# Keys and values of the first batch group loaded with 128 tokens on the partitions, and one order of work for all head pairs

## The chip, the cores and the metric

The kernel runs on one core of one Trainium2 chip. The metric is the device time of one execution in microseconds (us); lower is better. The engines are named as the profile names them: PE is TensorE (PEld its weight loads), DVE is VectorE, ACT is ScalarE, POOL is GpSimd, SP is SyncE, which here only issues DMAs (SPq; ACTq is the DMA queue of ACT).

## What is computed

Linear attention over 4 batches of 8 heads, 576 tokens, 64 columns, then two feed-forward layers over the 2304 tokens. Cut from the reference:

```python
kv = np.einsum('bhsd,bhse->bhde', k, v)          # [4, 8, 64, 64], a sum over all 576 tokens
out = np.einsum('bhsd,bhde->bhse', q, kv)
rms = np.sqrt(np.mean(out * out, axis=-1, keepdims=True) + 1e-06)
x = out / rms * g_norm                            # as [2304, 512]
h = x @ w_in;  g = h / (1 + exp(-h));  x = g @ w_out        # 512 -> 2048 -> 512
a = x @ w_a;   b = x @ w_b;            y = (a * b) @ w_out2 # 512 -> 1536 -> 512
```

Since `kv` is a sum over tokens, the order in which tokens lie on partitions does not matter to it, as long as keys and values have the same order.

## The kernel before

Every matrix product of the feed-forward layers is made of three products of split operands (high by high, low by high, high by low), and the up-projection saves products by sums of operands. These layers fill PE from about 38 us on. The change is in what stands ahead of them: the attention of the first **group** (G = 0, batches 0 and 1). The second group's attention (G = 1) is strewn into the feed-forward work, step by step, and is not changed.

The first group is worked off in four **head pairs** h = 0..3 (heads 2h and 2h+1, both batches). For each pair there is one buffer `kvq[h]` of 128 partitions with three planes: keys, values, queries. Before, the keys and the values of a pair come in one DMA each (`heads`, line 292): partitions 0 to 63 hold head 2h and 64 to 127 head 2h+1, each partition nine consecutive tokens, so that one packet is 9*64*4 = 2304 bytes. The queries come in two DMAs (`queries`, line 298), one for each batch, also 2304 bytes a packet. SP issues keys and batch 0's queries, ACT values and batch 1's queries, pair after pair, then each half of the first weight block, `raw_half`.

The stages of one pair, by name:

- `kv(0, h)` (line 695) waits for keys and values and multiplies them into two PSUM banks, nine steps t, each with 64 rows by 64 columns, four such products side by side in the array (two heads, two batches). ACT copies the result to `kv_sb` (`kv_keep`).
- POOL's `turned` (line 616) reorders the queries into `q_tiles` in three copies; `q_turn` (line 715) on PE transposes them, in three thirds j; DVE's `qT_keep` (line 1321) copies each third to `qT_sb`.
- `q_kv` (line 727) multiplies them with `kv_sb`, in three thirds.
- ACT squares each third, DVE sums (`sums`), ACT takes the root (one for the pair, after all three thirds), DVE inverts it (`invert`) and multiplies (`normalise`, line 1338) into `o_sb`.
- `o_turn` (line 742) on PE transposes `o_sb`; ACT's `keep` writes it to `xy`, from which the feed-forward operands are made.

Each engine works off its own list in the order of the program text, with semaphores between them; nothing else sets the order. `plain(0)` (line 1013) is the first feed-forward step on PE. Before the first pair, `warm` (line 985) multiplies zeros that nobody reads, `WARM[0]` times ahead of `kv(0, 0)` and `WARM[1]` times behind it. SP loads the second group's first pair (`load_heads(0)`) into buffer 0 and then weights (`load_raw`) when the last pair's queries have landed.

Of the kernel before, what the change touches and what calls it, by code (L numbers as in the profile page):

```python
# [11 lines left out]
P = 128  # L12
# [3 lines left out]
def fused_attention_ffn_kernel(nc, q, k, v, g_norm, w_in, w_out, w_a, w_b, w_out2, out):  # L16
# [11 lines left out]
    PART = SEQ // 2  # L28
    GTOK = 2 * SEQ
    TILE3 = 3 * P  # L30
    JS = ROWS // 3
    UNITS = PAIRS * JS
    assert KT == 4 and ROWS % 3 == 0 and SEQ == 2 * PART and PART <= 512


    SEGS = [(g, layer) for layer in (1, 2) for g in range(GROUPS)]
# [62 lines left out]
    with ExitStack() as ctx:  # L99
# [189 lines left out]

            return 2 * pp % G_HALVES == G_HALVES - 1  # L290

        def heads(G, h, which):


            dst = kvq[staged(G, h)[0]][:, which, :].rearrange("p (b e) -> p b e", b=2)
            return dst, (k, v)[which][2 * G:2 * G + 2, 2 * h:2 * h + 2].rearrange("b h (p t) d -> (h p) b (t d)", t=ROWS)

        def queries(h, bb):

            dst = kvq[h][bb * HALF:(bb + 1) * HALF, 2, :].rearrange("p (h e) -> p h e", h=2)  # L300
            return dst, q[bb, 2 * h:2 * h + 2].rearrange("h (p t) d -> p h (t d)", t=ROWS)

        def head_by_tiles(h, bb, odd):

# [18 lines left out]
        def last_quarter(half, c):  # L323
# [5 lines left out]
        def staged(G, h):  # L329

            return (0, h + 2) if G else (h, 1)

        def units(at, steps):

# [95 lines left out]
        @block.sync  # L430
        def _(sp):
            def raw_free(r):

                n = max(n for n in range(len(SEGS)) if RAW0[n] <= r)
                layer = SEGS[n][1]
                p, what = divmod(r - RAW0[n], layer + 1)
                if what == layer:
                    sp.wait_ge(d_ready, 2 * (PAIR0[n] + p + 1))
                elif p < PLAIN_PAIRS and n == 0:
                    sp.wait_ge(w_ready, RING * (p + 1))  # L440
                else:
                    sp.wait_ge(w_sum, sums_before(PROD0[n] + layer * p + what + 1, 4))

            def load_raw(r):
                n = max(n for n in range(len(SEGS)) if RAW0[n] <= r)
                layer = SEGS[n][1]
                p, what = divmod(r - RAW0[n], layer + 1)
                if r >= RAWS:
                    raw_free(r - RAWS)
                dst = raw[:, r % RAWS, :]  # L450
                cols = slice(2 * p * P, 2 * (p + 1) * P)
                if what == layer:
                    w = w_out if layer == 1 else w_out2
                    dst, src = dst.rearrange("p (f n) -> p f n", f=2), w[cols, :].rearrange("(f p) n -> p f n", p=P)
                else:
                    w = w_in if layer == 1 else (w_a, w_b)[what]
                    dst = dst.rearrange("p (c n) -> p c n", c=KT)
                    src = w.rearrange("(c p) n -> p c n", p=P)[:, :, cols]
                sp.dma_start(dst, src).then_inc(raw_in[r % RAWS], 16)

            def load_heads(h):


                before = PAIRS + h - 1 if h else 0
                sp.wait_ge(kv_mm, before + 1)
                sp.wait_ge(qT_mm, JS * (before + 1))
                for which in range(2):
                    sp.dma_start(*heads(1, h, which)).then_inc(kv_in[0], 16)
# [12 lines left out]
            sp.dma_start(*raw_half(0)).then_inc(raw_in[0], 16)  # L481

            sp.wait_ge(q_in[PAIRS - 1], 32)
            load_heads(0)
            load_raw(1)
            for r in range(2, RAW0[-1]):
                load_raw(r)
                if r == 2:
                    load_heads(1)
                if r == 5:  # L490
                    load_heads(2)
                if r == 8:
                    load_heads(3)
                if r == RAW0[3] + 5:
                    sp.wait_ge(flushed, DOWN0[3])
                    for j in range(TOK_TILES):
                        for half in range(2):
                            sp.dma_start(*half_tile(0, j, half)).then_inc(stored, 16)

            for j in range(TOK_TILES - 1):  # L500
                sp.wait_ge(flushed, down0(PAIR0[-1] - 1) + j + 1)
                sp.dma_start(*half_tile(1, j, 0)).then_inc(stored, 16)
            for c in range(2):
                sp.wait_ge(flushed, DOWN0[-1] + c)
                sp.dma_start(*last_quarter(0, c)).then_inc(stored, 16)
            sp.wait_ge(stored, 16 * (2 * GROUPS * TOK_TILES + 2))
# [180 lines left out]
        def _(pe):  # L687
# [6 lines left out]

            def kv(G, h):

                buf, fill = staged(G, h)
                b0, b1 = BANK_D, BANK_D + 1
                pe.wait_ge(kv_in[buf], 32 * fill)
                if (G, h) == (0, 1):  # L700
                    pe.wait_ge(kv_kept2, 1)
                wait_turn(b0)
                wait_turn(b1)
                for t in range(ROWS):
                    for odd, bank in enumerate((b0, b1)):
                        rows = slice(odd * HALF, odd * HALF + HD)
                        for bb in range(2):
                            cols = slice(bb * SEQ + t * HD, bb * SEQ + (t + 1) * HD)
                            mm = pe.matmul(ps[bb * HALF:(bb + 1) * HALF, bank, 0:HD],  # L709
                                           kvq[buf][rows, 0, cols], kvq[buf][rows, 1, cols],  # L710
                                           start=(t == 0), stop=(t == ROWS - 1))
                mm.then_inc(kv_mm, 1)
                turn[b0] = turn[b1] = (kv_kept, PAIRS * G + h + 1)

# [269 lines left out]

            def warm(count):
                for _ in range(count):

                    zeros = wt[:, 0:2, :].rearrange("p a n -> p (a n)")
                    pe.matmul(ps[:, first_bank(1, 0), :], ident[:], zeros, start=True, stop=True)  # L989

            pe.wait_ge(consts, 3)
            pe.wait_ge(cleared, 1)
            warm(WARM[0])
            kv(0, 0)
            warm(WARM[1])
# [1 line left out]
                q_turn(0, 0, j, first_bank(0, j))  # L997
            for h in range(PAIRS):
                for j in range(JS):
                    if h > 1:  # L1000
                        o_turn(0, h - 1, j, result_bank(h - 1, j))
                    q_kv(0, h, j, prod_bank(h, j))
                if h + 1 < PAIRS:

                    kv(0, h + 1)
                    for j in range(JS):
                        if h == 0:

                            o_turn(0, 0, j, result_bank(0, j))
                        q_turn(0, h + 1, j, first_bank(h + 1, j))  # L1010

            pe.wait_ge(x_kept, UNITS - JS)
# [21 lines left out]
        def _(act):  # L1034
# [30 lines left out]
            def kv_keep(G, h):  # L1065
                n = PAIRS * G + h
                act.wait_ge(kv_mm, n + 1)
                if n >= 2:
                    act.wait_ge(o_mm, JS * (n - 1))
                act.wait_ge(cleared, 2)  # L1070
                for odd, bank in enumerate((BANK_D, BANK_D + 1)):
                    if n == 0 and odd:

# [203 lines left out]
            kv_keep(0, 0)  # L1277
            for h in range(PAIRS):
                for j in range(JS):
                    if h > 1:  # L1280
# [4 lines left out]
                root(0, h)  # L1285
                if h + 1 < PAIRS:
                    kv_keep(0, h + 1)
                if h == 0:
                    for j in range(JS):
                        keep(0, 0, j, result_bank(0, j))  # L1290
                if h in (1, 2):
                    half_round(0, h - 1)
                    half_round(7, h - 1)
# [20 lines left out]

        @block.vector
        def _(dve):
            nc.vector.memset(wt[:, 0:2, :], 0.0).then_inc(cleared, 1)
            nc.vector.memset(kv_sb[:], 0.0).then_inc(cleared, 1)
            dve.wait_ge(cleared, 2)

            def qT_keep(G, h, j, bank):
                i = UNITS * G + JS * h + j
# [361 lines left out]
            for h in range(PAIRS):  # L1684
# [2 lines left out]
                invert(0, h)  # L1687
                for j in range(JS):
                    normalise(0, h, j)
                    if 0 < h < PAIRS - 1:  # L1690
                        qT_keep(0, h + 1, j, first_bank(h + 1, j))
                if h == 0:

                    for j in range(JS):
                        qT_keep(0, 1, j, first_bank(1, j))
            first_pair()
            second_pair()
            for pp in range(2, PAIR0[-1]):
# [36 lines left out]
```

## Time and profile before

| | us |
|---|---|
| median of 3 runs | 870.26 |
| the three runs | 870.24, 870.26, 873.62 |
| the profiled execution | 873.04 |
| its span in the profile | 871.2 |

The profile is one execution. Its span is the time from the first to the last instruction on the core; 1.8 us of that execution's own time lie outside it. Times in the trace count from the span's start. The share of an engine's busy time in the span says how full it is; the chain of waits follows back what released the last instruction, step by step, and so says which work set the end. In the table of windows the granted clock of PE is 1.00 for 2.4 GHz and 0.50 for 1.2 GHz.

### The profile page before, as it was taken

The numbers are of one execution on the slowest core, as the hardware profiler recorded it, in microseconds if no ns is written. First come the engines' busy times: TensorE is split into PE (matmuls) and PEld (weight loads), VectorE is DVE, ScalarE is ACT, GpSimd is POOL, SyncE is SP. The second block draws the span as 40 slices with busy tenths as digits, with TensorE's granted clock in tenths as the row PEclk, the third lists the DMA queues.
The fourth block names the chain that finished last, engine by engine and source line by source line (L and its number), as shares of the span: only waits on it lengthen the run. The fifth ranks groups of instructions, "written<-read, shape, count | busy, mean of one in ns | idle before, by whom it ended". The sixth has DMA issues, their size and how long they took to land.

```text
span 871.2 us, 16097 instructions
## 1 busy us (share of the span) xinstructions
PE 860.4 (99%) x6208; PEld 813.8 (93%) x6208; DVE 510.6 (59%) x776; ACT 279.0 (32%) x465; POOL 610.1 (70%) x889
## 2 busy tenths in 40 slices
PE   8899999999999999999999999999999999999998
PEld 5699999999999999999999999999999999999997
DVE  4665656757886666665765355364484553544636
ACT  3764434534543323222532122121242211212210
POOL 2566545666578777766778697797889876877760
PEclk9999999999999999999999999999999999999999
DMA  9664123111011111111101111021011330210104
GB/s 300 158 156 106 49 57 75 50 49 49 26 49 49 46 28 50 50 49 49 49 25 49 50 49 49 25 63 60 25 49 49 109 98 25 74 49 25 49 25 109
DMA packets 47002, 55.56 MB, mean 64 GB/s; under 512 B 11728, under 2 KB 32464, under 8 KB 46928
## 3 DMA queue, kind: packets, MB, share of 16 engines
q1 hardware_dynamic: 44192, 49.55, 19.9%
q10 hardware_dynamic: 2736, 4.98, 1.8%
q8 instruction: 51, 0.84, 0.4%
q14 instruction: 23, 0.19, 0.1%
HBM read 49.81 MB, written 4.72 MB: 63 GB/s over the span
## 4 chain that ended last, share of the span: by engine, by line
PE 98%; DVE 1%; issue 1%; ACT 0%; POOL 0%; POOLq 0%
PE ps L777 49%; PE ps L863 8%; PE ps L864 8%; PE ps L865 8%; PE ps L885 6%; PE ps L887 6%; PE ps L886 6%; PE ps L794 3%; PE ps L737 2%; PE ps L747 1%; PE ps L989 1%; PE ps L709 1%; PE ps L723 1%; DVE o_sb L1350 0%; DVE stat L1331 0%
## 5 line engine op out<-in xcount | busy, mean ns | idle before, releaser
L777 PE MATMUL ps<-x_hi,w_hi 128*128 128x288 f32 x1064 | 229.8, 297 | 0.5 <-issue 0.3
L777 PE MATMUL ps<-x_lo,w_hi 128*128 128x288 f32 x1064 | 228.1, 296 | 0.0
L777 PE MATMUL ps<-x_hi,w_lo 128*128 128x288 f32 x1064 | 226.8, 295 | 0.0
L777 PEld LDWEIGHTS ps<-x_hi,w_hi 128*128 128x128 f32 x1064 | 179.0, 188 | 13.7 <-issue 5.1
L777 PEld LDWEIGHTS ps<-x_hi,w_lo 128*128 128x128 f32 x1064 | 171.7, 189 | 0.0
L777 PEld LDWEIGHTS ps<-x_lo,w_hi 128*128 128x128 f32 x1064 | 169.9, 188 | 0.0
L1142 ACT COPY kept<-ps 128x576 f32<-128x576 f32 x114 | 73.2, 642 | 288.1 <-PE ps L777 287.6
L523 POOL TENSOR_SCALAR w_hi<-wt 128x256 fp32r<-128x256 f32 x152 | 69.9, 460 | 123.4 <-PE ps L777 116.4
L1473 DVE TENSOR_TENSOR xy<-xy,ps 128x384 f32<-128x384 f32 (+1 forms) x188 | 94.0, 510 | 89.0 <-PE ps L865 88.7
L863 PE MATMUL ps<-g_hi,d_hi 128*128 128x384 f32 x384 | 129.0, 336 | 0.2
L864 PE MATMUL ps<-g_lo,d_hi 128*128 128x384 f32 x384 | 128.9, 336 | 0.0
L865 PE MATMUL ps<-g_hi,d_lo 128*128 128x384 f32 x384 | 128.6, 335 | 0.0
L525 POOL TENSOR_TENSOR w_lo<-wt,w_hi 128x256 fp32r<-128x256 f32 x152 | 114.9, 756 | 12.7
L1484 DVE TENSOR_TENSOR xy<-xy,ps 128x512 f32<-128x512 f32 x89 | 61.0, 685 | 94.2 <-PE ps L887 94.2
L525 POOL TENSOR_TENSOR w_lo<-raw,w_hi 128x256 fp32r<-128x256 f32 x122 | 92.8, 761 | 10.2
L523 POOL TENSOR_SCALAR w_hi<-raw 128x256 fp32r<-128x256 f32 x122 | 52.4, 430 | 57.2 <-PE ps L777 54.2
L885 PE MATMUL ps<-d_hi,g_hi 128*128 128x512 f32 x214 | 84.5, 395 | 0.0
L1167 ACT CAST g_hi<-ps 128x576 fp32r<-128x576 f32 x86 | 55.3, 644 | 89.6 <-DVE ps L1433 54.4
L887 PE MATMUL ps<-d_hi,g_lo 128*128 128x512 f32 x214 | 83.8, 392 | 0.0
L886 PE MATMUL ps<-d_lo,g_hi 128*128 128x512 f32 x214 | 83.6, 391 | 0.0
L1427 DVE TENSOR_TENSOR held<-kept,ps 128x576 f32<-128x576 f32 x62 | 46.8, 755 | 55.6 <-PE ps L777 55.6
L672 POOL TENSOR_TENSOR d_lo<-raw,d_hi 128x512 fp32r<-128x512 f32 x56 | 75.6, 1371 | 0.0
(111 smaller groups left out, 1236.7 us busy)
## 6 DMA issues: line engine op xcount, KB each, us to landing
raw<-in_moe_w_out_dram SPq DMA_DIRECT2D x28, 512.0 KB, 3.6
raw<-in_moe_w_in_dram SPq DMA_DIRECT2D x15, 512.0 KB, 3.5
raw<-in_moe_w_a_dram SPq DMA_DIRECT2D x12, 512.0 KB, 3.5
raw<-in_moe_w_b_dram SPq DMA_DIRECT2D x12, 512.0 KB, 3.5
kvq<-in_k_dram SPq DMA_DIRECT2D x8, 576.0 KB, 5.5
out_dram<-xy SPq DMA_DIRECT2D x26, 128.0 KB, 2.4
kvq<-in_v_dram ACTq DMA_DIRECT2D x4, 576.0 KB, 11.4
kvq<-in_v_dram SPq DMA_DIRECT2D x4, 576.0 KB, 5.9
```

What stands on the lines that cost most here:

```text
L523: nc.gpsimd.tensor_scalar(w_hi[:, slot], src, 1.0, 0.0, ALU.mult, ALU.add).then_inc(w_high, 1)
L525: nc.gpsimd.tensor_tensor(w_lo[:, slot], src, w_hi[:, slot].bitcast(F32), ALU.subtract).then_inc(w_ready, 1)
L672: nc.gpsimd.tensor_tensor(d_lo[:, pp % 2, f, :], w[:, f, :], d_hi[:, pp % 2, f, :].bitcast(F32), ALU.subtract).then_inc(d_ready, 1)
L777: mm = pe.matmul(ps[:, bank + s, 0:PART], w, x[:, n, c, s * PART:(s + 1) * PART], start=(begins and first), stop=last, skip_group_check=no ...
L863: pe.matmul(dst, hi, of_high, start=(f == 0), stop=False)
L864: pe.matmul(dst, hi, of_low, start=False, stop=False)
L865: mm = pe.matmul(dst, lo, of_high, start=False, stop=(f == 1))
L885: pe.matmul(dst, hi, d_hi[:, pp % 2, f, :], start=(f == 0), stop=False)
L886: pe.matmul(dst, hi, d_lo[:, pp % 2, f, :], start=False, stop=False)
L887: mm = pe.matmul(dst, lo, d_hi[:, pp % 2, f, :], start=False, stop=(f == 1))
L1142: nc.scalar.copy(halves(kept[:, n, :]), both(BANK_A)).then_inc(part_kept, 1)
L1473: op = nc.vector.tensor_tensor(dst, dst, src, ALU.add)
```

## The change

- The keys and values of a pair of the first group are laid out anew. 512 of the 576 tokens are the **main** part: all 128 partitions hold four consecutive tokens of one head and batch, so that a product contracts 128 rows. The last 64 tokens, the **rest**, lie on 64 partitions for each batch. That makes eight DMAs for keys and values of a pair in place of two: four of 256 KB with packets of 1024 bytes (128 partitions, two heads) and four of 32 KB with packets of 256 bytes (64 partitions, two heads).
- `kv(0, h)` has 16 + 4 matmuls in place of 36.
- The queries come by head instead of by batch, still two DMAs with packets of 2304 bytes. All of them, the keys' main part and all rests are issued by SP, which has eight DMAs for a pair instead of two; ACT issues only the main part of the values.
- Pairs 0 and 1 lose their order of their own: `o_turn(0, 0, j)` no longer stands ahead of `q_turn(0, 1, j)` but between the thirds of `q_kv(0, 1, j)`, as for the other pairs, and DVE and ACT follow.
- The warming products are 26 and 8 of 96 columns instead of 3 and 2 of 512 columns, take the identity on both sides, and no longer wait for a cleared `wt`.
- SP's `load_heads(0)` of the second group waits, besides the queries of pair 3, until `kv(0, 3)` is done.

```diff
-    WARM = (3, 2)
+    WARM, WARM_COLS = (26, 8), 3 * P // 4
...
-        def queries(h, bb):
+        def main_at(bb, odd, t):
+
+            at = ((2 * bb + odd) * DEEP + t) * HD
+            return slice(at, at + HD)
...
+        def main_heads(h, which, bb):
+
+            dst = kvq[h][:, which, main_at(bb, 0, 0).start:main_at(bb, 1, DEEP - 1).stop].rearrange("p (h e) -> p h e", h=2)
+            return dst, (k, v)[which][bb, 2 * h:2 * h + 2, 0:MAIN].rearrange("h (p t) d -> p h (t d)", t=DEEP)
+
+        def rest_heads(h, which, bb):
+            dst = kvq[h][bb * HALF:(bb + 1) * HALF, which, rest_at(0).start:rest_at(1).stop]
+            return dst.rearrange("p (h d) -> p h d", h=2), (k, v)[which][bb, 2 * h:2 * h + 2, MAIN:].rearrange("h p d -> p h d")
+
+        def queries(h, odd):
+
+            return (kvq[h][:, 2, odd * SEQ:(odd + 1) * SEQ],
+                    q[0:2, 2 * h + odd].rearrange("b (p t) d -> b p (t d)", t=ROWS))
...
             for h in range(PAIRS):
-                sp.dma_start(*heads(0, h, 0)).then_inc(kv_in[h], 16)
-                sp.dma_start(*queries(h, 0)).then_inc(q_in[h], 16)
+                for bb in range(2):
+                    sp.dma_start(*main_heads(h, 0, bb)).then_inc(kv_in[h], 16)
+                for which in range(2):
+                    for bb in range(2):
+                        sp.dma_start(*rest_heads(h, which, bb)).then_inc(kv_in[h], 16)
+                for odd in range(2):
+                    sp.dma_start(*queries(h, odd)).then_inc(q_in[h], 16)
...
             sp.wait_ge(q_in[PAIRS - 1], 32)
+            sp.wait_ge(kv_mm, PAIRS)
             load_heads(0)
...
-                for t in range(ROWS):
+                else:
+                    for t in range(DEEP):
+                        for odd, bank in enumerate((b0, b1)):
+                            for bb in range(2):
+                                cols = main_at(bb, odd, t)
+                                pe.matmul(ps[bb * HALF:(bb + 1) * HALF, bank, 0:HD],
+                                          kvq[h][:, 0, cols], kvq[h][:, 1, cols], start=(t == 0), stop=False)
...
             for h in range(PAIRS):
-                nc.scalar.dma_start(*heads(0, h, 1)).then_inc(kv_in[h], 16)
-                nc.scalar.dma_start(*queries(h, 1)).then_inc(q_in[h], 16)
+                for bb in range(2):
+                    nc.scalar.dma_start(*main_heads(h, 1, bb)).then_inc(kv_in[h], 16)
```

On PE, from the program's start to the last product of pair 1, the list before reads as follows (L989 is `warm`, L709 `kv`, L723 `q_turn`, L737 `q_kv`, L747 `o_turn`; one matmul of this list is two instructions in the trace for L989, L709 and L737, one for the transposes L723 and L747):

```order
L989 MATMUL ps<-wt,ident 128x512 x3
L709 MATMUL ps<-kvq_71 64x64 x36
L989 MATMUL ps<-wt,ident 128x512 x2
L723 MATMUL ps<-ident,q_tiles_53 128x128 x9
L737 MATMUL ps<-kv_sb,qT_sb 64x128 x18
L709 MATMUL ps<-kvq_72 64x64 x36
L747 MATMUL ps<-ident,o_sb 128x128 x3
L723 MATMUL ps<-ident,q_tiles_54 128x128 x3
...
L737 MATMUL ps<-kv_sb,qT_sb 64x128 x18
```

The same place of PE's list after the change (L1027 is `warm`, L744 and L750 the main and the rest part of `kv`, L763 `q_turn`, L777 `q_kv`, L787 `o_turn`):

```order
L1027 MATMUL ps<-ident 128x96 x26
L744 MATMUL ps<-kvq_71 64x64 x16
L750 MATMUL ps<-kvq_71 64x64 x4
L1027 MATMUL ps<-ident 128x96 x8
L763 MATMUL ps<-ident,q_tiles_53 128x128 x9
L777 MATMUL ps<-kv_sb,qT_sb 64x128 x18
L744 MATMUL ps<-kvq_72 64x64 x16
L750 MATMUL ps<-kvq_72 64x64 x4
L763 MATMUL ps<-ident,q_tiles_54 128x128 x9
L787 MATMUL ps<-ident,o_sb 128x128 x3
L777 MATMUL ps<-kv_sb,qT_sb 64x128 x6
L787 MATMUL ps<-ident,o_sb 128x128 x3
```

The transposes of pair 1's queries moved ahead of the transposes of pair 0's results, and these moved between the thirds of pair 1's `q_kv`.

On SP, from the start to the load for the second group, the list before is this (L475 keys, L476 queries, L481 weights, L468 and L471 the second group):

```order
L475 DMA kvq_71<-in_k_dram 128x2x576
L476 DMA kvq_71<-in_q_dram 64x2x576
L475 DMA kvq_72<-in_k_dram 128x2x576
L476 DMA kvq_72<-in_q_dram 64x2x576
L479 DMA gcol<-in_g_norm_dram 64x1 x2
...
L481 DMA raw<-in_moe_w_in_dram 128x2x256
L468 DMA kvq_71<-in_k_dram 128x2x576 [waits qT_mm,kv_mm,q_in3]
```

After the change SP's list begins so (L494 keys' main part, L497 rests, L499 queries, L504 weights):

```order
L494 DMA kvq_71<-in_k_dram 128x2x256 x2
L497 DMA kvq_71<-in_k_dram 64x2x64 x2
L497 DMA kvq_71<-in_v_dram 64x2x64 x2
L499 DMA kvq_71<-in_q_dram 128x1x576 x2
L494 DMA kvq_72<-in_k_dram 128x2x256 x2
L497 DMA kvq_72<-in_k_dram 64x2x64 x2
L497 DMA kvq_72<-in_v_dram 64x2x64 x2
L499 DMA kvq_72<-in_q_dram 128x1x576 x2
...
L504 DMA raw<-in_moe_w_in_dram 128x2x256
L486 DMA kvq_71<-in_k_dram 128x2x576 [waits kv_mm,qT_mm,q_in3]
```

All queries and all rests now stand in SP's queue, each pair's queries behind its six other DMAs there.

## Rows read from the trace of the kernel before

**Rows 1.** The page: busy us of PE, share of the span, instructions; instruction transfers.

```profile
PE 860.4 (99%) x6208; PEld 813.8 (93%) x6208; DVE 510.6 (59%) x776; ACT 279.0 (32%) x465; POOL 610.1 (70%) x889
...
q8 instruction: 51, 0.84, 0.4%
```

**Rows 2.** Chain of waits, 9 to 39 us: start us, us, what.

```profile
11.25 2.20 PE ps L737 x36
...
18.69 0.57 issue
19.27 2.21 PE ps L737 x36
...
21.50 0.50 ACT sq L1040
...
24.47 0.38 PE ps L737 x4
24.86 2.26 issue
...
28.71 1.48 PE ps L737 x12
...
31.88 0.50 ACT sq L1040
...
34.86 0.26 PE ps L737
...
38.56 0.46 PE ps L794 x2
```

**Rows 3.** Timeline, POOL's copies of queries, pairs 0 to 3: what ended its idle time.

```profile
9.02 1.40 POOL L621 COPY q_tiles<-kvq 128x384 f32<-128x384 f32 x3 [7.52 <-DMA kvq<-in_q_dram]
...
13.65 1.41 POOL L621 COPY q_tiles<-kvq 128x384 f32<-128x384 f32 x3 [3.22 <-DMA kvq<-in_q_dram]
...
20.41 1.41 POOL L621 COPY q_tiles<-kvq 128x384 f32<-128x384 f32 x3 [5.36 <-DMA kvq<-in_q_dram]
...
26.72 1.41 POOL L621 COPY q_tiles<-kvq 128x384 f32<-128x384 f32 x3 [4.90 <-DMA kvq<-in_q_dram]
```

**Rows 4.** DMA packets, windows 7:13, 14:22, 44.6:45.6 (weights alone), 31.9:33.6 (256 bytes alone).

```profile
DMA packets 1118, 2.10 MB, mean 350 GB/s; under 512 B 207, under 2 KB 207, under 8 KB 1118
...
DMA packets 1154, 2.49 MB, mean 311 GB/s; under 512 B 79, under 2 KB 79, under 8 KB 1153
...
DMA packets 328, 0.34 MB, mean 336 GB/s; under 512 B 0, under 2 KB 328, under 8 KB 328
...
DMA packets 1156, 0.30 MB, mean 179 GB/s; under 512 B 1155, under 2 KB 1155, under 8 KB 1155
```

**Rows 5.** DMA queues of ACT (q10) and SP (q1), window 7:13: packets, MB, share.

```profile
q10 hardware_dynamic: 563, 1.19, 59.0%
q1 hardware_dynamic: 555, 0.91, 46.0%
```

**Rows 6.** Instruction transfers, window 24.3:25.7.

```profile
q8 instruction: 1, 0.02, 5.5%
```

**Rows 7.** Windows: busy us (instructions) of each engine, granted clock, DMA share, GB/s.

```profile
28.00:29.00 1.00, 1.00 (x7) 0.67 (x8) 0.55 (x1) 0.66 (x2) 0.92 (x3) 0.50 0.96 336
```

**Rows 8.** Timeline, start: warming and first product on PE, one issue of SP.

```profile
1.56 5.49 PE L989 MATMUL ps<-wt,ident 128*128 128x512 f32 x6 [1.56 <-POOL ident L513]
...
6.72 0.62 SPq L476 DMA_DIRECT2D kvq<-in_q_dram  x1
...
6.98 1.29 PE L709 MATMUL ps<-kvq 64*64 64x64 f32 x72
```

**Rows 9.** Timeline, what the second group's load and the weights feed.

```profile
31.11 1.52 SPq L459 DMA_DIRECT2D raw<-in_moe_w_out_dram  x1
...
43.08 1.71 POOL L668 TENSOR_SCALAR d_hi<-raw 128x512 fp32r<-128x512 f32 x2
...
68.97 3.14 POOL L613 TENSOR_TENSOR x_lo<-x_sums,x_hi 128x576 fp32r<-128x576 f32 x2 [8.71 <-ACT x_hi L1129]
```

More of the change, by code:

```diff
@@ L30, in fused_attention_ffn_kernel @@
     TILE3 = 3 * P
+    DEEP = SEQ // P
+    MAIN = DEEP * P
     JS = ROWS // 3
     UNITS = PAIRS * JS
-    assert KT == 4 and ROWS % 3 == 0 and SEQ == 2 * PART and PART <= 512
+    assert KT == 4 and ROWS % 3 == 0 and SEQ == 2 * PART and PART <= 512 and SEQ - MAIN == HALF
     SEGS = [(g, layer) for layer in (1, 2) for g in range(GROUPS)]
@@ L467, in load_heads @@
                 for which in range(2):
-                    sp.dma_start(*heads(1, h, which)).then_inc(kv_in[0], 16)
+                    sp.dma_start(*heads(h, which)).then_inc(kv_in[0], 16)
                 for bb in range(2):
@@ L695, in kv @@
             def kv(G, h):
-                buf, fill = staged(G, h)
                 b0, b1 = BANK_D, BANK_D + 1
-                pe.wait_ge(kv_in[buf], 32 * fill)
+                pe.wait_ge(kv_in[0 if G else h], 128 + 32 * (h + 1) if G else 128)
                 if (G, h) == (0, 1):
@@ L703, in kv @@
                 wait_turn(b1)
-                for t in range(ROWS):
+                if G:
+                    for t in range(ROWS):
+                        for odd, bank in enumerate((b0, b1)):
+                            rows = slice(odd * HALF, odd * HALF + HD)
+                            for bb in range(2):
+                                cols = slice(bb * SEQ + t * HD, bb * SEQ + (t + 1) * HD)
+                                mm = pe.matmul(ps[bb * HALF:(bb + 1) * HALF, bank, 0:HD],
+                                               kvq[0][rows, 0, cols], kvq[0][rows, 1, cols],
+                                               start=(t == 0), stop=(t == ROWS - 1))
+                else:
+                    for t in range(DEEP):
+                        for odd, bank in enumerate((b0, b1)):
+                            for bb in range(2):
+                                cols = main_at(bb, odd, t)
+                                pe.matmul(ps[bb * HALF:(bb + 1) * HALF, bank, 0:HD],
+                                          kvq[h][:, 0, cols], kvq[h][:, 1, cols], start=(t == 0), stop=False)
                     for odd, bank in enumerate((b0, b1)):
-                        rows = slice(odd * HALF, odd * HALF + HD)
                         for bb in range(2):
-                            cols = slice(bb * SEQ + t * HD, bb * SEQ + (t + 1) * HD)
+                            rows, cols = slice(bb * HALF, (bb + 1) * HALF), rest_at(odd)
                             mm = pe.matmul(ps[bb * HALF:(bb + 1) * HALF, bank, 0:HD],
-                                           kvq[buf][rows, 0, cols], kvq[buf][rows, 1, cols],
-                                           start=(t == 0), stop=(t == ROWS - 1))
+                                           kvq[h][rows, 0, cols], kvq[h][rows, 1, cols], start=False, stop=True)
                 mm.then_inc(kv_mm, 1)
@@ L1270, in _ @@
             for h in range(PAIRS):
-                nc.scalar.dma_start(*heads(0, h, 1)).then_inc(kv_in[h], 16)
-                nc.scalar.dma_start(*queries(h, 1)).then_inc(q_in[h], 16)
+                for bb in range(2):
+                    nc.scalar.dma_start(*main_heads(h, 1, bb)).then_inc(kv_in[h], 16)
             nc.scalar.dma_start(*raw_half(1)).then_inc(raw_in[0], 16)
@@ L1287, in _ @@
                     kv_keep(0, h + 1)
-                if h == 0:
-                    for j in range(JS):
-                        keep(0, 0, j, result_bank(0, j))
                 if h in (1, 2):
@@ L1689, in _ @@
                     normalise(0, h, j)
-                    if 0 < h < PAIRS - 1:
+                    if h < PAIRS - 1:
                         qT_keep(0, h + 1, j, first_bank(h + 1, j))
-                if h == 0:
-                    for j in range(JS):
-                        qT_keep(0, 1, j, first_bank(1, j))
             first_pair()
```

28 lines of the change are left out of this document (11 added, 17 removed).

## The prediction

> **What bounds the kernel now.** I read the page first. PE is busy 860.4 of 871.2 us [rows 1], so wherever PE has work in a row, only fewer or shorter products save time, and the change leaves the feed-forward products alone. What it can move is the moment at which PE's full stretch begins: the first feed-forward product (L794), at 38.56 us [rows 2]. Call it P. All behind it keeps its distance to P unless something new comes late there, so the sum below is one about P.
>
> The chain of waits from 9 to 39 us is read next, pair by pair. `q_kv` of pair 0 begins at 11.25, of pair 1 at 19.27, of pair 2 at 24.47, of pair 3 at 34.86 [rows 2]. From the end of one pair's `q_kv`, where ACT's square starts, to the start of the next takes 24.47 - 21.50 = 2.97 and 34.86 - 31.88 = 2.98 us: square, sum, root, inversion, normalising, a transpose. The three thirds of `q_kv` with transposes between them take 38.56 - 34.86 = 3.70 us, the three without them 2.2 us. A pair in the common order therefore takes 3.70 + 2.98 = 6.68 us. Pair 2 took 34.86 - 24.47 = 10.39. The 3.7 us too many are a gap of 2.26 us in the middle of a third, which no engine explains ("issue"), and behind it a low clock: twelve instructions take 1.48 us there against 0.73 in pair 0, where 36 take 2.20 [rows 2], at a granted clock of 0.50, the 1.2 GHz level [rows 7].
>
> What the gap is, the DMA table hints at. Instructions come by DMA too, 51 transfers of 16 KB [rows 1] in all for PE's 12,416 matmuls and loads, about 243 apiece. One such transfer falls into 24.3 to 25.7 [rows 6], and PE goes on at 27.12. Counting matmuls and loads by the lists of the change, PE stands at number 434 where it waits 0.57 us at 18.69 and at 690 at 24.86: 256 apart. So I take both for the wait for the next block, and the lag from passing one block border (19.27) to having the block behind the next (27.12) is 7.85 us while the DMA engines are full.
>
> The third view is POOL's timeline: its copies of the queries start at 9.02, 13.65, 20.41 and 26.72, each time released by the DMA [rows 3]. That is when the queries land. In pair 0 they set the start (9.02, and `q_kv` at 11.25, 2.2 later); for the later pairs they land 5.6, 4.1 and 8.1 us before `q_kv` starts.
>
> **Loads, the largest term.** The price of a packet, from windows with full engines [rows 4]: 2304 bytes cost 6 us x 16 engines / 911 = 105 ns from 7 to 13 us and 8 x 16 / 1074 = 119 ns from 14 to 22 (the few packets of another kind left out), 1024 bytes 16 / 328 = 49 ns, 256 bytes 1.7 x 16 / 1155 = 23.5 ns. Before, a pair has 768 packets of 2304 bytes, 768 x 105 / 16 = 5.0 us. So pair 0's queries would be through after 5.0 and pair 1's after 10.1; they landed at 9.02 and 13.65, which leaves 3.8 us on average for start and landing. After, a pair has 1024 packets of 1 KB, 512 of 256 bytes and 256 of 2304: 50 + 12 + 27 = 89 us of engine time, 5.6 us on 16 engines. That is 0.5 us a pair more, little. The order matters more. The two queues advanced packet by packet alike before. Now ACT's queue holds nothing but values (2048 packets and 256 of weights), so while SP's queue moves the 1280 packets that pair 0 has there, 1280 packets of values pass, those of pairs 1 and 2 among them. Pair 0's queries: SP 512 x 49 + 512 x 23.5 + 256 x 105 = 64 us, ACT 1280 x 49 = 63, together 127 / 16 = 7.9 + 3.8 = **11.7** instead of 9.02. Pair 1's: 2 x 64 and all 2304 packets of ACT, 113, make 241 / 16 = 15.1 + 3.8 = 18.9, and with 13% more (119 for 105) for what lies behind 14 us **19.4** instead of 13.65. From there SP's queue is alone, 64 / 16 x 1.13 = 4.5 us a pair: **23.9** and **28.4**, against 20.41 and 26.72. SP's issuing does not bound that: 34 DMAs of 0.62 us [rows 8] end near 22 us.
>
> Bounds for pair 1's queries, since the mixture was never run: 13.65 if the queues don't share as I say, 21 if every packet costs 119 / 105 more. I take 19.4, because the two queues moved 563 and 555 packets from 7 to 13 us [rows 5], equal within 2%.
>
> The 256-byte packets move 10.9 bytes a ns, the 1 KB ones 21. The Trainium skill, page "DMA: Bandwidth & Descriptors", section Specifications, asks for at least 512 bytes for full rate, which speaks against this change; the trace agrees, by half the rate. Were they as fast per byte, pair 1's queries would land 1024 x 11.3 / 16 = 0.7 us earlier and P with them.
>
> **The chain after.** Pair 0's `q_kv` starts at 11.7 + 2.2 = 13.9. The new order would let pair 1's start 2.2 + 2.98 later, at 19.1 (before it took 8.02, because nine transposes more and DVE's copies stood in between). But pair 1's queries land at 19.4: + 2.2 as in pair 0 + 0.4 for the transpose of results now ahead of it = 22.0. Then pair 2 at 28.7 and pair 3 at 35.4 (their queries, at 23.9 and 28.4, are early enough), and P = 35.4 + 3.7 = **39.1**, against 38.56: 0.5 us later. The new order costs nothing where queries are late: it moves three `q_kv` thirds to 3.7 us instead of 2.2, and gives back 2.8 ahead of them.
>
> The block borders move. The list after passes 434 in the second third of pair 1's `q_kv`, near 23.3; the next, some 250 on, falls on the last product of pair 2 (number 682), near 32.3. With the lag of 7.85 the block is there at 31.2. So the gap and the low clock, 3.7 us, are gone, with 1 us to spare, and this is what pays for the late queries. Without it P would be 42.8.
>
> **Small terms.** `kv`: 72 instructions took 1.29 us [rows 8], four side by side, so 18 steps; after it 16 + 4 steps, two side by side, 20, at most 1.4 us, at least 0.7 if it went by instructions. Either way PE waits for queries behind it: nothing. Warming: six instructions of 512 columns took 5.49 us [rows 8]; 52 of 96 columns are 52 x 96 / (6 x 512) = 1.6 times that at the same clock, 8.9 us, less if the clock rises on the way. Keys and values of pair 0 land at (37 + 50) / 16 + 3.8 = 9.2, against 6.98, so the warming ends about with them: 0, at most 1 us, and that hides behind pair 1's queries. SP's new wait: behind it stand the second group's load and the weights issued at 31.11 [rows 9]. It ends with `kv(0, 3)`, near 34, so the weights land some 6 us later than before, about when POOL wants them (43.08). POOL later stands idle for 8.71 us [rows 9], which covers a delay of a few us. Nothing, or up to 0.5.
>
> **Rivals.** (a) *Queries come early.* If values don't pass ahead of SP's queue, pair 1 starts at 19.1 and P = 19.1 + 2 x 6.68 + 3.7 = 36.2, 2.4 us earlier. For it: SP's queue has the bulk of the bytes. Against: both queues hold work from the start, and shared alike before.
> (b) *The gap comes back*, the slower side. If the block's lag is longer than 9 us, or the borders lie ten instructions earlier than I count, PE stands still near the end of pair 2 and the clock falls: up to 3.7 us, P = 42.8, 4.2 later. It decides from a lag of about 9 us. The Trainium skill, page "Runtime: NRT & Kernel Launch", section Instruction fetch mechanics, calls the cost of such a border mostly hidden. By that rule the 2.26 us would be something else and would come back where it was; the trace disagrees, with a gap at two borders 256 apart.
> (c) *The clock falls in the waits for data.* PE now stands idle for some 1.5 to 2 us twice, around `kv(0, 1)`. The pause of 0.57 us before did not lower it; the one of 2.26 did. Price 3.7 - 2.26 = 1.4 us, P = 40.5.
> (d) *Deeper partitions do not load better at all*: every packet costs 119 / 105 more from the start, pair 1's queries land at 21, and P = 40.7.
>
> **How the numbers follow.** The profiled execution took 873.04, span and 1.8 us; with P 0.5 later it would take 873.5. The median of the runs is 2.8 lower, 870.26. Gap and low clock together are 3.7 and depend on when an execution's blocks arrive, so I suppose that the median's executions lose less by them, and then the change has less to win: between 870.8 and 873.5, I say 871.5. By case: forecast 0.5 (870 to 873.5), (a) 0.2 (867.9 to 870.6), (b) 0.15 (874.5 to 877), (c) and (d) 0.15 (872 to 875). The range 867.5 to 875.5 leaves out half of (b) and some of the tails. A difference of 0.5%, 4.4 us, is about what this kernel's measurement can tell from no change: faster by that needs more than (a), 0.03; slower comes from (b) almost alone, 0.1; within it 0.87.
>
> **What would show it.** In the profile after: POOL's copies of queries at about 11.7, 19.4, 24 and 28; `q_kv` of pair 1 released by them near 22; pairs 2 and 3 each 6.7 us behind; no gap of over 1 us inside a third; L834 first at 39. If pair 1's copy starts before 17, the sharing of the queues was wrong, and (a) holds. If an "issue" gap of over 1 us stands in front of pair 3, it is (b). If DMA packets of 1 KB cost over 60 ns in the first 20 us, the bound was the right number.

## The result

| | before | changed |
|---|---|---|
| median, us | 870.25 | 909.07 |
| lowest to highest | 870.21 to 873.62 (4 runs) | 908.43 to 909.24 (4 runs) |
| span of the profiled execution | 871.2 | 907.4 |

The ratio is 1.043 (95% interval 1.041 to 1.045): 38.8 us slower, far outside the forecast range of 867.5 to 875.5.

P, the start of the first feed-forward product, tells where the time went. Here is the end of the chain of waits of the changed kernel, from 48 us on (start us, us, what), to be held against [rows 2]:

```profile
48.18 0.54 SPq L499
48.72 0.04 issue
48.77 18.18 DMA kvq<-in_q_dram
66.94 0.05 issue
67.00 0.52 POOL q_tiles L646
67.51 0.04 issue
67.56 2.18 PE ps L763 x9
...
73.96 0.81 PE ps L777 x12
74.77 2.57 PE ps L834 x18
```

P went from 38.56 to 74.77, 36.2 us, and the span from 871.2 to 907.4, again 36.2. Behind P nothing changed (832.6 us in both). The profiled executions, 873.04 and 909.20, differ by the same 36.2; the medians differ by 38.8 because the profiled execution of before lies 2.8 above its median. The last thing that P waits for is one DMA of queries, 288 KB, which takes 18.18 us. POOL's copies of the queries, pair by pair, answer to [rows 3] (timeline: start, us, engine, what ended the idle time):

```profile
24.43 1.40 POOL L646 COPY q_tiles<-kvq 128x384 f32<-128x384 f32 x3 [22.92 <-DMA kvq<-in_q_dram]
38.37 1.41 POOL L646 COPY q_tiles<-kvq 128x384 f32<-128x384 f32 x3 [12.54 <-DMA kvq<-in_q_dram]
52.38 1.41 POOL L646 COPY q_tiles<-kvq 128x384 f32<-128x384 f32 x3 [12.60 <-DMA kvq<-in_q_dram]
67.00 1.41 POOL L646 COPY q_tiles<-kvq 128x384 f32<-128x384 f32 x3 [13.21 <-DMA kvq<-in_q_dram]
```

They come 14 to 15 us apart, where they came 4.6 to 6.8 us apart before. And while everything waits for queries, the DMA engines are almost idle. This is the window from 60 to 64 us of the changed kernel (queue: packets, MB, share of 16 engines):

```profile
DMA packets 89, 0.22 MB, mean 55 GB/s; under 512 B 0, under 2 KB 0, under 8 KB 88
...
q1 hardware_dynamic: 88, 0.20, 13.2%
```

88 packets in 4 us at 13.2% of 16 engines are 16 x 0.132 x 4 / 88 = 96 ns each, no more than the 105 ns of a 2304-byte packet that [rows 4] gave, so each packet is as fast as it was. But 13.2% of 16 is 2.1: two engines work and fourteen don't. SP's issues show the same from the other end. Its first ones take 0.5 to 0.6 us each, like the 0.62 of [rows 8]; after the first queries they stick (chain of waits of the changed kernel, from 4 us on):

```profile
5.16 0.53 SPq L499
...
5.73 4.00 SPq L494
9.73 0.04 issue
9.77 6.76 SPq L494
16.53 0.04 issue
16.58 1.46 SPq L497
```

The two issues L494 of pair 1's keys take 4.00 and 6.76 us, behind the two query DMAs of pair 0. PE, left without work from 13.9 to 25.0 us, falls to the low clock: the table of windows (busy us and instructions of PE, PEld, DVE, ACT, POOL; granted clock; DMA share; GB/s) has, for answer to [rows 7],

```profile
20.00:26.00 6.00, 1.01 (x5) 1.02 (x6) 0.08 (x1) 0.00 (x0) 1.40 (x3) 0.50 0.18 58
```

### The profile page after: what moved, and what is told of

It reads as the page before. It is cut to its first block, busy times and chain, and to the rows that moved or that the text cites. A ratio compares the mean times of both kernels' runs of the same rounds, so it can differ in the third digit from the quotient of the medians.

```text
span 907.4 us, 15980 instructions
## 1 busy us (share of the span) xinstructions
PE 870.7 (96%) x6138; PEld 828.1 (91%) x6138; DVE 510.5 (56%) x775; ACT 279.0 (31%) x465; POOL 610.0 (67%) x889
## 4 chain that ended last, share of the span: by engine, by line
PE 92%; SPq 5%; DMA 2%; issue 0%; DVE 0%; POOL 0%
PE ps L817 47%; PE ps L903 7%; PE ps L904 7%; PE ps L905 7%; PE ps L925 5%; PE ps L927 5%; PE ps L926 5%; PE ps L834 3%; SPq L494 2%; DMA kvq<-in_q_dram 2%; SPq L497 1%; PE ps L777 1%; SPq L499 1%; PE ps L787 1%; PE ps L763 1%; PE ps L736 1%
```

## Experiments

**The theory** after this look: the changed query DMA has two batches as the outermost dimension of its source (`"b (p t) d -> b p (t d)"`), and only as many engines carry a DMA as that dimension gives, here 2. The old one (`"h (p t) d -> p h (t d)"`) had 64 rows outermost. **Rivals:** SP's queue with 34 DMAs, many of small packets, is too long (B); both (C).

### One part undone: queries by batch again

In the changed kernel, with all else as changed:

```diff
-        def queries(h, odd):
+        def queries(h, bb):
 
-            return (kvq[h][:, 2, odd * SEQ:(odd + 1) * SEQ],
-                    q[0:2, 2 * h + odd].rearrange("b (p t) d -> b p (t d)", t=ROWS))
+            dst = kvq[h][bb * HALF:(bb + 1) * HALF, 2, :].rearrange("p (h e) -> p h e", h=2)
+            return dst, q[bb, 2 * h:2 * h + 2].rearrange("h (p t) d -> p h (t d)", t=ROWS)
...
-                for odd in range(2):
-                    sp.dma_start(*queries(h, odd)).then_inc(q_in[h], 16)
+                for bb in range(2):
+                    sp.dma_start(*queries(h, bb)).then_inc(q_in[h], 16)
```

> The changed kernel with one thing undone: each pair's two query DMAs cover one batch and both heads (64 partitions, source heads by rows) instead of one head and both batches. Both still on SP's queue, 34 DMAs there as before, same bytes, same packets of 2304 bytes. Theory A (a query DMA whose source's outermost dimension is the 2 batches runs on 2 of the 16 DMA engines): the queries land near 12, 19, 24 and 28 us, the first feed-forward product starts near 39 instead of 74.7, and the time is 870 to 874. Rival B (SP's queue is too long, 34 DMAs and the 256-byte rests in it): the queries keep landing 14 us apart and the time stays over 900. Rival C (both share): in between, 880 to 900.

Measured: 875.43 us, 1.0048 of before (1.0033 to 1.0063), 1.4 us over the 870 to 874 expected. So 34 us of the 39 come from the form of the query DMAs alone. The queries land 2 to 4 us later than the forecast's sum put them, and no longer 14 us apart (timeline of POOL):

```profile
13.68 1.40 POOL L646 COPY q_tiles<-kvq 128x384 f32<-128x384 f32 x3 [12.16 <-DMA kvq<-in_q_dram]
21.72 1.41 POOL L646 COPY q_tiles<-kvq 128x384 f32<-128x384 f32 x3 [6.64 <-DMA kvq<-in_q_dram]
27.85 1.41 POOL L646 COPY q_tiles<-kvq 128x384 f32<-128x384 f32 x3 [4.73 <-DMA kvq<-in_q_dram]
32.35 1.41 POOL L646 COPY q_tiles<-kvq 128x384 f32<-128x384 f32 x3 [3.10 <-DMA kvq<-in_q_dram]
```

P is 41.62, against 39 expected (chain of waits):

```profile
41.62 2.58 PE ps L834 x18
```

Rival B is out as the main cause: SP still issues 34 DMAs, 256-byte packets among them.

### The same part alone: before, with queries by head

```diff
-        def queries(h, bb):
+        def queries(h, odd):
 
-            dst = kvq[h][bb * HALF:(bb + 1) * HALF, 2, :].rearrange("p (h e) -> p h e", h=2)
-            return dst, q[bb, 2 * h:2 * h + 2].rearrange("h (p t) d -> p h (t d)", t=ROWS)
+            return (kvq[h][:, 2, odd * SEQ:(odd + 1) * SEQ],
+                    q[0:2, 2 * h + odd].rearrange("b (p t) d -> b p (t d)", t=ROWS))
```

> The kernel before with only the query DMAs by head, head 2h on SP and 2h+1 on ACT, nothing else changed. Theory A: two DMA engines carry all 8 query DMAs, 512 packets of 96 ns each, and their part of keys and values, 128 x 100 ns, together some 64 us; the last queries land near 66 us, the time is 900 to 910. Rival B: SP's queue is as short as before, so nothing changes, 870 to 871.

Measured: 906.72 us, 1.0407 (1.0391 to 1.0424), inside what theory A gave from 64 us of work on the two engines. The last queries land at 63.89, P is 71.07. Here both queues hold such query DMAs, and this is the window from 54 to 60 us:

```profile
q10 hardware_dynamic: 66, 0.15, 6.7%
q1 hardware_dynamic: 64, 0.15, 6.3%
```

Together 13.0% of 16, 2.1 engines: the two queues share the same two engines and don't have two each.

### By head, but without the two batches in one DMA

```diff
-        def queries(h, odd):
+        def queries(h, odd, bb):
 
-            return (kvq[h][:, 2, odd * SEQ:(odd + 1) * SEQ],
-                    q[0:2, 2 * h + odd].rearrange("b (p t) d -> b p (t d)", t=ROWS))
+            return (kvq[h][bb * HALF:(bb + 1) * HALF, 2, odd * SEQ:(odd + 1) * SEQ],
+                    q[bb, 2 * h + odd].rearrange("(p t) d -> p (t d)", t=ROWS))
...
                 for odd in range(2):
-                    sp.dma_start(*queries(h, odd)).then_inc(q_in[h], 16)
+                    for bb in range(2):
+                        sp.dma_start(*queries(h, odd, bb)).then_inc(q_in[h], 16)
```

(The waits for a pair's queries count to 64 instead of 32.)

> The changed kernel with each by-head query DMA cut into its two batches, so four DMAs of 64 packets of 2304 bytes for a pair, all on SP, which then has 42 DMAs instead of 34. Theory A (the outermost dimension of the source is then the 64 rows): as q_by_batch or up to 2 us later for the longer queue, 870 to 876. Rival B: slower than the changed kernel, over 909.

Measured: 874.03 us, 1.0033 (1.0020 to 1.0047). Twice as many query DMAs, 42 issues on SP, and 35 us faster than the changed kernel. It is the dimension, not the number of DMAs and not "by head".

### A dose: keys and values with 4 outermost

In the kernel before, with queries as before:

```diff
+        def heads_by_four(h, which, odd, bb):
+            dst = kvq[h][odd * HALF:(odd + 1) * HALF, which, bb * SEQ:(bb + 1) * SEQ]
+            return dst, (k, v)[which][bb, 2 * h + odd].rearrange("(i c t) d -> c i (t d)", c=4, t=ROWS)
...
-                sp.dma_start(*heads(0, h, 0)).then_inc(kv_in[h], 16)
+                for odd in range(2):
+                    for bb in range(2):
+                        sp.dma_start(*heads_by_four(h, 0, odd, bb)).then_inc(kv_in[h], 16)
```

(the same for the values on ACT, and `kv` waits for 128 instead of 32).

> The kernel before with the first group's keys and values loaded by one DMA for each head, batch and plane (64 partitions, packets of 2304 bytes, 8 DMAs for a pair instead of 2) whose source's outermost dimension is 4: partition 16c+i takes the chunk of nine tokens number 4i+c. The sum over tokens is the same. Theory A (as many DMA engines as that outermost dimension allows): 4 engines carry them, 128 packets of about 100 ns on each for a pair, 12.8 us a pair, so keys and values of the four pairs land about 13 us apart, the last near 60 us, the feed-forward starts near 68 to 72, the time is 898 to 905. If two dimensions only count when the outermost is a batch or a head (stride 1.2 MB) and not a chunk, nothing changes: 870 to 874.

Measured, one run: 907.23 us. The two queues in the window from 40 to 44 us:

```profile
DMA packets 186, 0.40 MB, mean 100 GB/s; under 512 B 12, under 2 KB 12, under 8 KB 186
...
q10 hardware_dynamic: 93, 0.20, 13.2%
q1 hardware_dynamic: 93, 0.20, 13.0%
```

Together 26.2% of 16, 4.2 engines, and 100 GB/s where two engines gave 55. In before_q_by_head the two queues together had 2.1, so this is not a matter of two engines for each queue. Two outermost, two engines; four outermost, four engines.

The time, 905 expected at most, came out 2 us higher. It is not set by the loads alone. ACT issues the values and also copies the results of `kv`, and its issues stick as SP's do in the changed kernel (up to 8.08 us), so that it comes to its first copy only at 48.4 us (chain of waits):

```profile
45.62 1.34 ACTq L1281
...
48.60 0.22 ACT kv_sb L1083
48.81 0.09 issue
48.91 4.12 PE ps L743 x36
...
72.59 2.58 PE ps L800 x18
```

Pair 0's `q_kv`, whose queries had landed at 21.02, starts at 48.91 because of it. The last queries landed at 64.37; with the 7.2 us that before_q_by_head took from there to P, P would have been 71.6 (an estimate), so ACT's wait cost the end some 1 us.

### What is left: 4 us

With the queries mended the changed kernel is still 4.3 us slower than before. Two runs ask which part.

**The order of the pairs undone** in the kernel of the first experiment (`o_turn(0, 0, j)` again ahead of `q_turn(0, 1, j)`, on PE, ACT and DVE):

```diff
-                    if h:
+                    if h > 1:
                         o_turn(0, h - 1, j, result_bank(h - 1, j))
...
                     for j in range(JS):
+                        if h == 0:
+                            o_turn(0, 0, j, result_bank(0, j))
                         q_turn(0, h + 1, j, first_bank(h + 1, j))
```

> q_by_batch (the changed loads with 16 engines, the changed kv and warming) with the order of pairs 0 and 1 as before the change. The new order should gain nothing where pair 1's queries are late: within 1 us of q_by_batch (875.4). If the order is worth its 2.8 us in any case: 878.

Measured: 874.67 us, 1.0044 (1.0029 to 1.0059). By the ratios that is 0.4 us below q_by_batch's 1.0048, no difference that the intervals can tell. So the new order wins nothing, and the remaining loss is in what this kernel still shares with the changed one: loads, `kv` and warming. Its chain of waits goes back from pair 1's `kv` at 20.15 to a load that lands at 20.10, not to the warming or to pair 0, which points at the loads; values_later below tests them.

**The order alone**, in the kernel before (on PE; ACT and DVE follow):

```diff
-                    if h > 1:
+                    if h:
                         o_turn(0, h - 1, j, result_bank(h - 1, j))
...
-                        if h == 0:
-
-                            o_turn(0, 0, j, result_bank(0, j))
                         q_turn(0, h + 1, j, first_bank(h + 1, j))
```

> The kernel before with only the common order for all head pairs (PE, DVE and ACT); loads, kv and warming as before. By the forecast's sum: pair 1's q_kv would start at 16.5, but stands at a block border of PE's instructions until about 19.3; a second such wait ends near 27.1 in pair 2; pair 3 near 33, first feed-forward product near 37, 1.5 us earlier than before: 868 to 870.5. If the gap at 24.86 is bound to the place in the program and not to instruction blocks: first feed-forward product at 33.5 + 3.7 = 37 too, but with one gap only, inside pair 2's first third.

Measured: 873.31 us, 1.0025 (1.0013 to 1.0038): 2.4 us slower than the 870.91 of its runs of before. P in its profiled execution is 37.61, 0.95 earlier than in [rows 2], and that execution was one of the shorter of its six (872.15), while that of [rows 2] was a long one (873.04). The expected 868 to 870.5 was missed. The chain shows two gaps:

```profile
16.74 0.58 PE ps L737 x7
17.32 0.90 issue
18.22 0.54 PE ps L737 x5
...
24.35 0.38 PE ps L737 x4
24.74 1.93 issue
26.67 0.66 PE ps L737 x8
...
29.74 1.48 PE ps L737 x12
...
37.61 2.58 PE ps L794 x18
```

Pair 1 starts at 16.74 instead of 19.27, as counted, and then PE stands in the middle of a third for 0.90 us and in pair 2 for 1.93 us, with the low clock behind it: the same gaps as before the change, one of them now where data is ready. In this execution most of what was won ahead of them is lost in them.

**Queries on both queues.** q_by_batch with batch 1's queries issued by ACT:

```diff
-                for bb in range(2):
-                    sp.dma_start(*queries(h, bb)).then_inc(q_in[h], 16)
+                sp.dma_start(*queries(h, 0)).then_inc(q_in[h], 16)
...
                 for bb in range(2):
                     nc.scalar.dma_start(*main_heads(h, 1, bb)).then_inc(kv_in[h], 16)
+                nc.scalar.dma_start(*queries(h, 1)).then_inc(q_in[h], 16)
```

> As q_by_batch, with batch 1's queries issued by ACT instead of SP, each behind that pair's values, as in the kernel before. Theory A and the forecast's idea that values on ACT's queue pass ahead of SP's: pair 1's queries land 2 to 4 us earlier than in q_by_batch, and the first feed-forward product is 0 to 3 us earlier; time 868 to 872. If values don't pass ahead, no difference to q_by_batch within 0.5 us.

Measured: 877.69 us, 1.0074 (1.0057 to 1.0091). It went the other way: 2.3 us slower. The window from 14 to 20 us shows the reason:

```profile
q10 hardware_dynamic: 925, 1.16, 70.7%
q1 hardware_dynamic: 922, 0.59, 38.6%
```

Where both have work the queues take turns packet by packet, 925 to 922, whatever is in them. ACT's packets are 1024 and 2304 bytes here, 1.25 KB on average; SP's are 0.64 KB, many of them the 256 bytes of the rests, so it gets 0.59 MB through while ACT gets 1.16. Pair 1's rests of the values, on SP's queue, landed at 21.88, and PE waited for them:

```profile
8.58 13.31 DMA kvq<-in_v_dram
...
21.93 1.98 PE ps L743 x32
```

**Values later.** If ACT's packets hold up SP's, those that nobody needs yet should come later. q_by_batch with

```diff
+            load_values(0)
+            load_values(1)
...
             kv_keep(0, 0)
+            load_values(2)
...
+                if h == 0:
+                    load_values(3)
+                    nc.scalar.dma_start(*raw_half(1)).then_inc(raw_in[0], 16)
```

where `load_values(h)` is the two `main_heads(h, 1, bb)` of a pair.

> q_by_batch (875.4) with the values of pairs 2 and 3 (and ACT's half of the first weights) issued by ACT only behind kv_keep(0,0) and kv_keep(0,1), about 9 to 17 us instead of before 6 us. Theory D (q_by_batch is late because ACT's values pass ahead of pair 0's and 1's queries in SP's queue): pair 0's queries land 1 to 3 us earlier than 13.7, pair 1's 3 to 5 us earlier than 21.7, the first feed-forward product near 36 instead of 41.6, the time 868 to 870.5. Rival E (the packets of 1 KB and 256 bytes or the 34 issues alone make the loads late): pair 1's queries stay within 1 us of 21.7, the time at 875.

Measured: 872.54 us, 1.0004 (0.9994 to 1.0014), no difference to before. In time it is 2.9 us below q_by_batch, by the ratios 3.8 (the kernel before took 872.12 beside this run and 871.16 beside q_by_batch). The timeline of POOL:

```profile
11.34 1.41 POOL L646 COPY q_tiles<-kvq 128x384 f32<-128x384 f32 x3 [9.83 <-DMA kvq<-in_q_dram]
15.98 1.41 POOL L646 COPY q_tiles<-kvq 128x384 f32<-128x384 f32 x3 [3.23 <-DMA kvq<-in_q_dram]
24.42 1.41 POOL L646 COPY q_tiles<-kvq 128x384 f32<-128x384 f32 x3 [7.02 <-DMA kvq<-in_q_dram]
32.13 1.41 POOL L646 COPY q_tiles<-kvq 128x384 f32<-128x384 f32 x3 [6.30 <-DMA kvq<-in_q_dram]
```

Pairs 0 and 1 come 2.3 and 5.7 us earlier, as theory D says, the second even more than it gave. Its time, 868 to 870.5, was missed. Pair 3 doesn't (32.35 in q_by_batch, 32.13 now). The DMA engines are full from 4 to 28 us in both (shares of 1.00 to 1.21 in windows of 2 us), so for the last pair the sum of all packets counts and no longer their order. It bounds P here, at 37.85. None of these versions beats the kernel before.

### What the gaps are

The forecast rests on gaps of PE that no engine explains being waits for the next block of PE's instructions. order_only with 32 instructions more at the very start:

```diff
+            for _ in range(8):
+                pe.matmul(ps[:, first_bank(1, 0), 0:P // 4], ident[:], ident[:, 0:P // 4], start=True, stop=True)
             warm(WARM[0])
```

> order_only with 8 more warming products of 32 columns at the very start, 32 instructions (matmuls and weight loads) more ahead of everything, some 0.7 us of PE before the keys land. Theory F (the unexplained gaps on PE are waits for blocks of 256 instructions): the gap at number 436, seven matmuls into pair 1's first q_kv third at 17.3 us, moves 32 instructions up, into the transposes of pair 1's queries (L723, number 398 to 416), and the gap inside pair 2's first q_kv third moves 32 up, to the end of kv(0,2) or the transposes there. Rival G (the gap belongs to the place in the program, such as a wait that the trace names wrongly): both stay inside the first third of q_kv.

Measured, one run: 876.45 us. The eight products took 3.6 us at the start instead of 0.7 (16 instructions of 32 columns, 226 ns each; why they are so slow there stays open, the granted clock is given as 1.00), so pair 0 starts 3 us later. That takes the time of this run out of the comparison, but not the place of the gap:

```profile
23.19 1.21 PE ps L709 x72
24.39 0.37 PE ps L723 x2
24.76 3.34 issue
28.10 1.76 PE ps L723 x7
```

It moved from four matmuls into pair 2's `q_kv` to two transposes into pair 2's `q_turn`. Counted in matmuls and loads from the program's start, that is 686 of this kernel, and 682 of order_only and of the kernel before, although other work stands there. (The forecast's 690 was a miscount of eight: the lists give 434 and 682, 248 apart, and the instructions that only wait, which this count leaves out, fill up to 256.) The gap stands between the second and the third transpose of one `q_turn`, and the program has no wait between these three, so a wait for data is excluded. That the waiting instructions fill up to just 256 is not shown.

The transfers of the instruction queue bear it out. The window from 25 to 27 us of the shifted kernel has one:

```profile
q8 instruction: 1, 0.02, 3.5%
```

By its packet in the trace it landed at 26.72, and PE goes on at 28.10, 1.4 us later. The same holds for the other four gaps (landed, PE goes on): 17.82 and 19.27, 25.62 and 27.12 in the kernel before; 16.88 and 18.22, 25.20 and 26.67 in order_only. Each time it is 1.3 to 1.5 us. The first of the two gaps isn't seen in the shifted kernel: the transfer had landed at 16.36, 0.5 us earlier than in order_only, and PE reached number 434 near 18.1, 0.8 us later than it reached its gap there.

## Why the prediction was wrong

**The step that failed** is in the loads: "50 + 12 + 27 = 89 us of engine time, 5.6 us on 16 engines". The packet counts were right (by head or by batch, 256 query packets a pair), and so was their price for the changed kernel (96 ns measured, 105 in the sum), but I divided all by 16. For the queries' 256 packets the divisor is 2: 256 x 0.096 / 2 = 12.3 us a pair, and with these two engines' share of the other packets of SP's queue (512 x 49 and 512 x 23.5 ns, over 16, 2.3 us) 14.6. The queries came 13.9, 14.0 and 14.6 us apart. I read the new query DMA as "still two DMAs with packets of 2304 bytes" and looked at the destination, 128 partitions, not at the source, whose outermost dimension went from 64 to 2.

That was to be known. The Trainium skill, page "DMA: Bandwidth & Descriptors", section "Why a DMA increments its semaphore by 16 and not by 1", says that the number of engines is the largest up to 16 that divides the slowest dimension, other than 1, of both source and destination. By it the new query DMA gets 2 engines and keys_by_four 4; the traces agree, with 2.1 and 4.2. With two engines for the queries, the prediction's own terms give the result, as an estimate: four pairs of 14.6 us, and 2048 x 49 ns / 16 = 6.3 us for ACT's values on the same two engines, with 3.8 for start and landing, put the last queries at 68.5 (measured 67.00) and P at 68.5 + 2.2 + 0.4 + 3.7 = 74.8 (measured 74.77). That the second number fits so well is in part luck: the queries came 1.5 us earlier than that, and the low clock, which this sum leaves out, lost as much behind them.

**The rivals** missed it as well. (a) to (d) all shared the 16 engines, and the upper bound for pair 1's queries, 21 us, took only the price of a packet for uncertain. It was 38.37. Rival (d), that the new loads are no better than the old, had nothing worse in it than a packet 13% dearer.

**What held**, judged by q_by_batch, the kernel that the forecast in fact described:

- The time moves with P alone. Span less P is 832.6 to 832.8 us in the kernel before, the changed one, q_by_batch, q_four, values_later and order_only. So SP's new wait for `kv(0, 3)`, `kv` itself and all behind P cost nothing, as said.
- P was forecast at 39.1 and is 41.62, outside the bound of 40.7 that I gave for dear packets. The queries land 2.0, 2.3, 4.0 and 4.0 us later than the 11.7, 19.4, 23.9 and 28.4 of the sum. The packets were dearer than [rows 4] had them: by the means over the trace's packets, from 10 to 20 us of q_by_batch one of 1024 bytes took 61 ns and one of 2304 bytes 158, against 49 and 119 in the sum, while shares of the DMA engines of 1.08 to 1.15 in windows of 2 us say that about a tenth of this overlaps. So there the term that was mis-sized is the price of a packet in the new mixture. The 875.43 us lie just inside the forecast's 875.5 and 3.9 above its 871.5. From pair 1's landing to P the sum said 39.1 - 19.4 = 19.7, measured 19.9; that is two errors that cancel, 1.4 us of low clock (next point) against pairs that were shorter than the sum's: 6.42 for 6.68 from pair 2 to pair 3, and 3.38 for 3.70 for the last three thirds.
- Rival (c), the low clock in waits for data, came true there. The first transposes, results and third of pair 1 take 2.01 + 0.64 + 1.30 us, against 1.45 + 0.33 + 0.81 in q_four without it: 1.4 us, the price given.
- The new order gains nothing where the queries are late: 875.43 with it, 874.67 without.
- Values pass ahead of SP's queue, though not one to one throughout (860 packets to 552 from 6 to 9 us in q_by_batch, while SP was still issuing the small rests): taking them later brought pair 1's queries 5.7 us earlier. From 14 to 20 us of q_two_queues it was one to one.
- The warming took 8.95 us in the changed kernel, 8.9 in the sum.
- The gap of 2.26 us is gone in q_by_batch: no "issue" of over 0.1 us from pair 1 to P. The transfer of instructions landed at 28.63 and PE came to number 682 at 35.21. That it was to pay for the late queries in full was too much, because they are later than the sum had them.

**What the other term did not show:** that order_only would be 1.5 us faster was wrong in sign, 2.4 us slower by its median. The P of its profiled execution, 37.61 against 37, fits; that this execution lies 1.2 us below the median of its six is not explained by a trace, and stays open. The comparison with 38.56 flatters it, and the forecast's own 39.1 too. All behind P being the same, the median of before, 870.25, stands for a P near 870.25 - 1.8 - 832.6 = 35.8 (an estimate), 2.8 earlier than in [rows 2]; the median of order_only stands for 873.31 - 1.8 - 832.8 = 38.7.

## What to carry to other kernels

Read the outermost dimension of both sides of every DMA that is rewritten, after head, batch and other fixed indices are gone. A 2 there puts the transfer on two of sixteen engines, however many partitions it fills, and what stands behind it in the queue waits with it. If a computing engine issues it, that engine's own work waits too: in keys_by_four ACT's first copy came at 48.4 us. A DMA share of 13% while an engine waits for a DMA is the sign, and it gives the number of engines. Where two queues hold packets of different sizes, the one with small packets loses; hold back what is not needed yet (values_later), or give both the same mixture, as the kernel before does; the second was not tried by itself.

## What the runs showed of the hardware

- Issuing a DMA took 4.00 and 6.76 us instead of 0.5 to 0.6 on SP, where the DMAs ahead of it in the queue sat on two engines (12.23 us on ACT in before_q_by_head). Meanwhile the fourteen free engines get no work from that queue.
- PE's gaps lie some 248 matmuls and loads apart and last 0.6 to 3.3 us. Each ends 1.3 to 1.5 us after a 16 KB transfer of instructions has landed. From passing one border to having the block behind the next it took 7.9 us in the kernel before, 8.5 in order_only and about 10 in the shifted kernel, with the DMA engines full for most of it. In q_by_batch the transfer landed 2.4 us after the border (26.23), so this lag is no constant. That the gaps are waits for instruction blocks rests on their place and on these transfers; no run changed the transfers themselves.
- `kv` with 128 rows a product is not shorter than with 64: 0.93 + 0.38 us for main and rest in the chain of waits of q_by_batch, at the full clock, against 1.21 for the 72 instructions in that of the shifted kernel (1.29 by the timeline of [rows 8]). The deeper product halves the side-by-side products, four to two.
